# Two gated MLPs on split products: seven products of halves instead of eight, in 768-token blocks, with the attention ahead of them

## The reference

```python
kv = einsum('bhsd,bhse->bhde', k, v)
out = einsum('bhsd,bhde->bhse', q, kv)
x0 = out / sqrt(mean(out * out, -1) + 1e-6) * g_norm      # heads side by side: 4608 x 512
x1 = (sigmoid(x0 @ w_gate) * (x0 @ w_val)) @ w_out
g  = x1 @ w2_gate
x2 = (g * sigmoid(g) * (x1 @ w2_val)) @ w2_out
```

## Time and profile before

| | |
|---|---|
| median of 3 runs | 1911.14 us (1910.02 to 1912.25) |
| the profiled execution, first to last instruction (its only recorded time) | 1909.4 us |
| TensorE busy | 1888.7 us, 99% |
| TensorE weight loads | 1563.7 us, 82% |
| VectorE, ScalarE, GpSimd busy | 534.8, 422.7, 164.0 us |
| moved by DMA | 130.32 MB, 68 GB/s on average |

### The profile page before, as it was taken

How to read it: one execution, slowest core, us unless ns; L and a number is a source line. 1 busy time by engine, 2 the same in 40 slices (tenths; PEclk the granted TensorE clock), 3 DMA queues, 4 the chain that set the end, 5 groups by cost and what they waited for, 6 DMA issues and landing times.

```text
span 1909.4 us, 23973 instructions
## 1 busy us (share of the span) xinstructions
PE 1888.7 (99%) x9312; PEld 1563.7 (82%) x9312; DVE 534.8 (28%) x852; ACT 422.7 (22%) x752; POOL 164.0 (9%) x110
## 2 busy tenths in 40 slices
PE   7999999999999999999999999999999999999999
PEld 6888888888888888888888888888888888888887
DVE  3333323233332323321212222222222222222222
ACT  4332222222222222211232111111111111111111
POOL 3540000000000000000242000000000000000000
PEclk8999999999999999999999999999999999999999
DMA  7653232232323213120343010101010101010000
GB/s 188 168 154 93 81 101 87 80 105 87 93 74 106 87 65 121 70 89 0 121 125 128 1 66 0 66 0 66 0 66 0 66 0 66 0 58 8 22 0 22
DMA packets 122996, 130.32 MB, mean 68 GB/s; under 512 B 43616, under 2 KB 80480, under 8 KB 122976
## 3 DMA queue, kind: packets, MB, share of 16 engines
q1 hardware_dynamic: 122976, 130.05, 21.6%
HBM read 82.84 MB, written 45.09 MB: 67 GB/s over the span
## 4 chain that ended last, share of the span: by engine, by line
PE 96%; DVE 1%; DMA 1%; ACT 1%; POOL 1%; issue 0%; SPq 0%; ACTq 0%; DVEq 0%
PE bank L392 60%; PE bank L413 30%; PE bank L375 2%; PE bank L347 1%; PE bank L365 1%; PE bank L385 1%; POOL rrms L750 0%; DVE ssum L644 0%; DMA w_stage<-in_moe_w_out_dram 0%; DMA q_sb<-in_q_dram 0%; DVE x_s L662 0%; ACT sq_xn L513 0%; DMA w_stage<-in_moe_w_gate_dram 0%; ACT wo_s L498 0%; DMA x_split<-o_flat 0%
## 5 line engine op out<-in xcount | busy, mean ns | idle before, releaser
L392 PE MATMUL bank<-x_s,wg_s 128*128 x2592 | 633.5, 393 | 1.3 <-DVE sig L673 0.7
L392 PE MATMUL bank<-x_s,wv_s 128*128 x2592 | 630.4, 391 | 0.0
L392 PEld LDWEIGHTS bank<-x_s,wg_s 128*128 128x128 f32 x2592 | 483.3, 188 | 102.0 <-DVE sig L673 1.2
L392 PEld LDWEIGHTS bank<-x_s,wv_s 128*128 128x128 f32 x2592 | 482.5, 188 | 98.2
L676 DVE TENSOR_TENSOR bank<-bank,sig 128x512 f32<-128x512 f32 x216 | 150.7, 698 | 505.3 <-PE bank L392 505.3
L530 ACT ACTIVATE sig<-bank 128x512 f32<-128x512 f32 x216 | 129.2, 598 | 607.6 <-PE bank L392 607.6
L534 ACT ACTIVATE gv_hi<-bank 128x512 fp32r<-128x512 f32 x216 | 129.1, 598 | 606.8 <-DVE bank L676 605.8
L413 PE MATMUL bank<-gv_hi,wo_s 128*128 128x512 f32 x864 | 213.4, 389 | 0.0
L413 PE MATMUL bank<-wo_s,gv_hi 128*128 128x512 f32 x864 | 213.4, 389 | 0.0
L680 DVE TENSOR_TENSOR gv_lo<-bank,gv_hi 128x512 fp32r<-128x512 f32 x216 | 149.3, 691 | 195.5 <-ACT gv_hi L534 195.5
L413 PEld LDWEIGHTS bank<-gv_hi,wo_s 128*128 128x128 f32 x864 | 162.2, 188 | 33.6
(11 more groups left out here) (39 smaller groups left out, 528.8 us busy)
## 6 DMA issues: line engine op xcount, KB each, us to landing
x_s<-x_split SPq DMA_DIRECT2D x32, 1024.0 KB, 6.6
x_split<-xT SPq DMA_DIRECT2D x28, 576.0 KB, 3.3
x_split<-o_flat SPq DMA_DIRECT2D x27, 512.0 KB, 3.1
q_sb<-in_q_dram SPq DMA_DIRECT2D x64, 144.0 KB, 3.0
out_dram<-o_flat SPq DMA_DIRECT2D x36, 256.0 KB, 2.2
k_sb<-in_k_dram SPq DMA_DIRECT2D x30, 288.0 KB, 3.6
v_sb<-in_v_dram SPq DMA_DIRECT2D x30, 288.0 KB, 4.1
w_stage<-in_moe_w_gate_dram SPq DMA_DIRECT2D x24, 256.0 KB, 3.0
```

Of the source, the lines that this page charges most:

```text
L392: mm = pe.matmul(dst[:], w[:, wp, kc, fj], x_at(tile, xp, kc), start=(kc == 0 and n == 0), stop=(kc == KC - 1 and n == 2))
```

## The change

Each MLP product of two matrices is cut into halves by halves, and the eight products of quarters are replaced by the seven of Strassen's scheme (in Winograd's form), on operands split in two parts as before. Products 1, 2, 3, ... 7 have sums and differences of quarters as operands: for x (S1 = a21 + a22, S3 = a11 - a21, S2 = S1 - a11, S4 = a12 - S2), for the weights likewise, formed by GpSimd. The quarters are: two halves of 384 tokens by two halves of d_model (or of d_ff), and two halves of d_model by two of d_ff.

The work is laid out anew. A block has 768 tokens, 6 blocks in all; each layer takes three passes over thirds of d_ff, and each pass goes over all blocks: 36 block-passes (`QN`). A block-pass has three windows: two up windows (gate and value of 128 features of each half of d_ff) and one down window (w_out). A window has 14 slots, (product, side), in the order of `ORDER`; side is gate or value in the up windows, the two 128-row pieces of an output half in the down window. A slot has 6 matmuls of 384 columns: 2 pieces of the contraction by 3 products of parts. The weights of one pass, as operands with high and low parts, lie in SBUF; six weight units of 1792 columns are formed and split at each change of pass. The x operands are formed in the first pass of a layer, stored to DRAM (7 x 768 KB a block), and loaded again in the other two passes. Partial results of a pass are stored (4 x 384 KB a block), loaded and added to in the next. In the down window the hidden operands H11, S1 and so on, formed by VectorE and GpSimd, are split into `hop`.

All 32 attention units run ahead of the MLPs, with banks of their own for four units, and store x0 unsplit and transposed. The second MLP's output is transposed too now, so each block is turned back at the end by 8 x 4 TensorE transposes, placed behind slots of the next block (`TURN_AT`), for the last block at the end of the kernel.

The diff, cut to what the prediction speaks of; only added lines are shown, since the whole function is replaced:

```diff
+ORDER = ((1, 0), (1, 1), (5, 0), (5, 1), (6, 0), (6, 1), (2, 0), (7, 0), (2, 1), (7, 1), (4, 0), (3, 0), (4, 1), (3, 1))
+WINDOWS = 3
+HOPS = ((1, 0), (5, 0), (2, 0), (6, 0), (1, 1), (5, 1), (6, 1), (2, 1), (7, None), (4, None), (3, None))
...
+    HN = 384
+    BLK = 2 * HN
+    NB = N // BLK
+    NPASS = 3
+    QN = 2 * NPASS * NB
...
+        W_STEP = {3 + 4 * i: i for i in range(6)}
+        X_STEP = {14 + 2 * i: pr for i, pr in enumerate(X_ORDER)}
+        STEPS = UNITS + 2
...
+            def load_xo(qq, pr):
+                l, p, blk = place(qq)
+                sp.wait_ge(slot_done, n_slot(qq - 1, 1, pr, 1))
+                sp.wait_ge(xo_stored[pr - 1], 16 * NB * (l + 1))
+                sp.dma_start(xo[:, pr - 1].bitcast(F32).rearrange("p a c n -> p (a c n)"), xod[l, blk, pr - 1]
+                             ).then_inc(xo_loaded[pr - 1], 16)
...
+            pe.wait_ge(ident_ready, 1)
+            for t in range(STEPS):
+                if t < UNITS:
+                    unit_kv(t)
+                    unit_qT(t, 0)
+                if 1 <= t <= UNITS:
+                    unit_o(t - 1)
+                if t < UNITS:
+                    unit_qT(t, 1)
+                if t >= 2:
+                    unit_xT(t - 2)
+
+            def turn(qq, i):
...
+                for d in range(KC):
+                    mm = pe.transpose(ps[0:SP_, 6 + i % 2, d * P:(d + 1) * P], res[:, t, d // 2, d % 2, at:at + SP_], ident[:])
+                mm.then_inc(turned, 1)
...
+                    for s, (pr, side) in enumerate(ORDER):
...
+                        elif pr == 6:
+                            pe.wait_ge(copied, n_copied(qq, w, 1, side))
+                        elif pr == 7:
+                            pe.wait_ge(copied, n_copied(qq, w, 6, side))
+                        elif pr == 4:
+                            pe.wait_ge(copied, n_copied(qq, w, 7, side))
...
+                        elif pr == 3:
+                            pe.wait_ge(summed, n_summed(qq, w, 22, side))
...
+                        for c in range(2):
+                            if w == 2 and side == 0:
+                                if pr in (7, 4, 3):
+                                    if c == 0:
+                                        pe.wait_ge(hop_lo, n_hop(qq, pr, None))
+                                else:
+                                    pe.wait_ge(hop_lo, n_hop(qq, pr, c))
+                            for i, (wp, xp) in enumerate(((HI, HI), (HI, LO), (LO, HI))):
+                                if w < 2:
+                                    lhsT = wa[:, w, side, W_AT[pr], wp, c * P:(c + 1) * P]
+                                    rhs = xo[:, pr - 1, xp, c, :]
+                                else:
+                                    lhsT = wb[:, c, W_AT[pr], wp, side * P:(side + 1) * P]
+                                    rhs = hop[:, HOP_SLOT[pr], xp, c, :]
...
+                        if qq > 0 and last_result(qq - 1) and (w, s) in TURN_AT:
+                            turn(qq - 1, TURN_AT[w, s])
...
+            for t in range(STEPS):
+                if t < UNITS:
+                    unit_kv(t)
+                if t >= 2:
+                    unit_scale(t - 2)
+                if 1 <= t <= UNITS:
+                    unit_norm(t - 1)
+                if t in W_STEP:
+                    split_w(W_STEP[t])
+                if t in X_STEP:
+                    split_x(0, X_STEP[t])
...
+                def hop_split(pr, c):
+                    dve.wait_ge(hop_hi, n_hop(qq, pr, c))
+                    nc.vector.tensor_tensor(hop_place(pr, c, LO), hop_source(pr, c), hop_place(pr, c, HI).bitcast(F32),
+                                            ALU.subtract).then_inc(hop_lo, 1)
...
+                        hidden(22)
+                        if l == 1:
+                            silu(21)
+                        total(12, 0)
+                        if w == 1:
+                            hop_split(1, 1)
+                        hidden(21)
+                        total(12, 1)
+                        if l == 1:
+                            silu(12)
+                        hidden(12)
+                        if w == 0:
+                            hop_split(1, 0)
+                    else:
+                        hop_split(5, 1)
+                        hop_split(6, 1)
+                        hop_split(2, 1)
+                        hop_split(7, None)
...
+                def hidden_s(c):
+
+                    pool.wait_ge(h_done, n_hid(qq, c, 21))
+                    if c == 0 and qq > 0:
+                        pool.wait_ge(hop_lo, len(HOPS) * qq)
+                    nc.gpsimd.tensor_tensor(s14[:, c], h21[:, c], h22[:, c], ALU.add).then_inc(s_made, 1)
+                    pool.wait_ge(s_made, n_s(qq, (S1_0, S1_1)[c]))
+                    nc.gpsimd.tensor_tensor(h21[:, c], h11[:, c], h21[:, c], ALU.subtract).then_inc(s_made, 1)
+                    pool.wait_ge(hop_lo, n_hop(qq, 1, c))
+                    pool.wait_ge(s_made, n_s(qq, (S3_0, S3_1)[c]))
+                    nc.gpsimd.tensor_tensor(h11[:, c], s14[:, c], h11[:, c], ALU.subtract).then_inc(s_made, 1)
...
+                nc.gpsimd.tensor_tensor(s14, h12, h11, ALU.subtract).then_inc(s_made, 1)
```

1336 lines of the change are left out of this document (756 added, 580 removed).

## The result

The changed kernel takes 2049.28 us (median of 4 runs, 2045.84 to 2050.8) and the kernel before, run beside it, 1911.64 us: the ratio is 1.0718, with a 95% interval of 1.0703 to 1.0734. The prediction was 1836 us, faster with 0.81. It was wrong in the sign, by 213 us.

A forecast was written before the change was run, and what follows sets the result against it. TensorE was taken as the bound. Attention 192, matmuls 1551, turns 17, hand-over 29, pass changes with x splits 29 and tail 16 gave 1834, plus 1.7: 1836 us; range 1795 to 1880, all bounds 1741 to 1947.

The forecast's parts named there:

- rival 5: MLPs: x operands arrive late, TensorE waits in each pass; 61 us more, 1897 us; chance 0.05.
- rival 4: MLP matmuls: each waits for its weight load, 188 ns apart; 1706 us for them, total 1991 us; chance 0.07.
- The 83 ns of the transposes: MLP matmuls: transposes loading 128 weight columns each follow 83 ns apart, so weight loads fit well inside 171 ns.
- I take 171: MLP matmuls: pace of 171 ns per 384-column matmul, chosen between 170.0 and 173.4; 1551 us for 9072.
- Nearly as their columns: MLP matmuls: 128-column matmuls 107 ns and 96-column transposes 83 ns apart, read as pace going nearly by columns.
- the rates of stretches with the DMA engines full: Attention up front: 48 MB move at 235 to 297 GB/s, taking 162 to 204 us; 182 was taken.
- Rival 3: Attention up front: runs at the earlier prologue's pace, half clock included, 229 us; total 1873 us; chance 0.12.
- the ring: Attention: VectorE's scale waits for GpSimd's power, the next norm behind scale; 4.64 us a unit, 158 us for 34.
- With spares this thin I take half, 0.8 each: Hand-over from second up window to down window: 0.8 us wait each, 29 us over 36, between bounds 0 and 61.
- Rival 1: Hand-over to the down window: VectorE and GpSimd exclude each other, 61 us instead of 29, total 1868 us; chance 0.28.
- 5 us each, 25: Five changes of pass: VectorE's weight splits of 2.1 us lie ahead of hand-over and down slots; 5 us each, 25.
- some 0.3 us in 12 blocks, 4: x preparation: the split of x ahead of the last down product costs some 0.3 us in 12 blocks, 4 us.

The follow-up runs named there:

- m1: Separate measuring kernel, computing nothing of the reference: TensorE split matmuls of four widths, VectorE and GpSimd additions alone and beside each other; no total time given.
- e4: Changed kernel plus eight dense 128-column products, results unread, in each of the 32 attention steps; 2044.54 us, ratio 1.0697.
- e8: e7 plus four dense products in each attention step; 1897.38 us, ratio 0.9927.
- e2: Changed kernel with all seven sums of hidden operands of a block-pass on VectorE instead of GpSimd; 1948.5 us, ratio 1.0197.
- e1: Changed kernel with GpSimd's x sums S1 and S3 placed after the first up window's hidden sums, not ahead; 2018.89 us, ratio 1.0567.
- e3: Changed kernel without loading, forming and splitting of weights after the first pass, so the output is wrong; 1947.9 us, ratio 1.019.
- e5: e2 with two weight units loaded a block earlier and the weight splits spread over up windows, none in a down window; 1917.29 us, ratio 1.0029.
- e7: e5 with x operand 5's split in the down window, two next-pass weight units formed earlier, x operand 2 split after the last hidden split; 1905.25 us, ratio 0.9963.
- e9: e8 with SyncE issuing loads of two next-pass weight units ahead of the stores of x operands 1 and 5; 1894.4 us, ratio 0.99.
- m2: Separate measuring kernel, computing nothing of the reference: transposes back to back, and short product bursts with gaps, to see what lowers TensorE's clock; no total time given.

## Why the prediction was wrong

**What held.** The number of matmuls, the turns (18 for 17) and the tail (15 for 16) came out. The operand loads are hidden (rival 5 false): every wait of TensorE in a steady block is released by VectorE's split, none by a load. That holds for TensorE's own operands; the raw x and the weights come late to GpSimd, see below. A weight load is no bound at 384 columns (rival 4 false): 173.3 is under 188, and in m1 matmuls with a full 128 x 128 load each come 110 ns apart. "The 83 ns of the transposes" was a slightly better case than that.

**The pace.** "I take 171" should have been the other bound, 173.4. The two narrow rows that were to choose between the bounds, 107 ns at 128 columns and 83 at 96, do not lie on the line through the wide ones (m1: 227, 173, 120 ns at 512, 384, 256). "Nearly as their columns" compared them with each other only: per column they cost 0.84 and 0.86 ns, the 512-column product 0.44, so they could not choose between its bounds. 21 us.

**Attention.** 47 MB moved in 212 us: the volume of the forecast (48 MB) at 222 GB/s. The failed step is, as far as is known, the rate: "the rates of stretches with the DMA engines full" were read as those of the whole, and the forecast took a middle of 162 to 204 us where the engines' share is only 0.82 on average. 26 us. Rival 3 (229 us, a unit every 6.59 us, the half clock included) was the nearer one: the half clock was there, and the norms come every 6.36 us. Products that keep TensorE at work bring 5 us net in e4 and 8 in e8, from which the clock's own price does not follow. Whether the transfers, the half clock or the loads' own waits set the pace of the long steps stays open; the ring alone is shorter, since norms come 4.4 us apart in the fastest steps.

**The hand-over.** "With spares this thin I take half, 0.8 each" failed: it is 1.57 and 2.0 us, 64 us, where the bound by exclusion was 1.7 and 61. Rival 1 was right in mechanism, place and price: L861 and L906 lengthened (1.35 of the 1.56 us by the estimate under e2), the wait released by VectorE's split. The nearest rows could not show it, since VectorE's operations there read PSUM and at most one buffer, the form that m1 finds untouched. That was noticed in the prediction; averaging the two cases instead of deciding by the form of the instructions was the mistake. 35 us.

**The changes of pass and x preparation.** Here lies the sign: 155 us where "5 us each, 25" and "some 0.3 us in 12 blocks, 4" were set. Both sentences count VectorE's splits alone, and those were priced well (2.1 us each; 2.08 in e2). The step left out is what stands in GpSimd's and ScalarE's queues. On GpSimd the wait for the x transfer (4.1 us in block-pass 2), the x sums (3.7 us) and at a change of pass eight weight differences (5.7 us) stand ahead of the first half's hidden sum S1; the prediction followed only the second half's. ScalarE is in order too, so its split waits for GpSimd and a copy out of PSUM waits for the split, and TensorE stops in the second up window, one window before the place that was examined. At a change of pass ScalarE's weight splits wait for GpSimd's differences as well, and hold up the same copies without any hidden sum. On top comes the lower clock after such waits, which no term had.

How much each is worth: e1 moves the x sums and takes 30 us. e3 removes all work on the weights and takes 97 us off the block-passes. e2 frees the hidden sums from GpSimd's queue, and of its 96 us only some 40 belong here, the other 56 to the hand-over. So the chain through the hidden sum is the smaller part of the 155 us; the larger is the weights' own loading, forming and splitting, of which e5 to e7 win back 40 us by placing them elsewhere (89 us above steady blocks in e2, 49 in e7).

**The sum.** 26 + 21 + 35 + 126 = 208 of the 210 us by which the span missed. With the terms as measured the removed eighth of the matmuls (1763 to 1572 us, 191 us) is outweighed (324 against 191) by 72 us of attention run alone beyond the 147 us that all but the MLP matmuls took before, and by 18 + 64 + 155 + 15 us of turns, waits and tail. The scheme itself is no loss: e9 has the same matmuls and is 1% faster than the kernel before.

## What to carry to other kernels

When work is added to an engine with an in-order queue, list for each piece what stands behind it on that engine, and what stands behind the instruction that waits for it on the next one: a queue at 37% of its time held up TensorE at two removes. Price VectorE against GpSimd by the form of the operands, not by average load: with two SBUF inputs beside a GpSimd instruction each waits for the other (1.29 us a pair where GpSimd alone needs 1.1, and VectorE's 0.56 grown to 1.1 to 1.35 on the path). Here it paid to put the short sums of the critical hand-over on the engine whose next instructions need them. A block-pass that takes exactly its matmuls (43.68 us here) is the reference against which every other block's loss can be read off.

## What the runs showed of the hardware that was not expected

- A 384-column addition on GpSimd takes 1.01 us alone, on VectorE 0.56; beside each other with SBUF operands 1.21 and 1.25 (m1).
- The pace of split products is columns/2.4 + 13 ns at 512, 384 and 256 columns (227, 173, 120), but 110 ns at 128 columns (m1).
- TensorE's level can fall without a long stop: after three bursts of 0.92 us with 1.33 us between them it fell to 1.2 GHz (m2). In the changed kernel it fell for short stretches behind waits of TensorE, in which 384-column products come 320 ns apart instead of 173. The clock column shows 1.00 also where the trace has no clock record (the attention of the changed kernel, whose transposes come 160 ns apart instead of 83); the distance of like instructions is the safer reading.
- The same attention program ended at 210.4 us in one execution and at 218.1 in another (e8, e9).
